# Slots of 384 rows instead of 256, one block of the first layer per PSUM bank in a ring of three, sum of mixture 2 and weight splits behind the fifth block

## What is computed

```python
out = np.einsum('hk,bskhg->bshg', w, x_unf)      # causal 7-tap average per head
# mixture 1: every token goes to its best expert of 8
expert_idx = np.argmax(x @ w_gate, axis=1)
for e in range(E):
    mask = expert_idx == e
    h = np.maximum(x[mask] @ w1[e], 0.0)         # 192 -> 1024
    out[mask] = gate_w[mask, None] * (h @ w2[e]) # 1024 -> 192
# mixture 2: noisy logits, every token goes to two experts of 8
noisy_logits = logits + np.log1p(np.exp(x @ w_noise)) * noise
top2 = np.argpartition(-noisy_logits, 2, axis=1)[:, :2]
for e in range(E):
    for k in range(2):
        mask = top2[:, k] == e
        out[mask] += top2_w[mask, k, None] * (np.maximum(x[mask] @ w1[e], 0.0) @ w2[e])
```

## Time and profile before

| | us |
|---|---|
| median of 3 runs | 2036.11 (2036.06 to 2037.99) |
| the profiled execution, its own time | 2038.28 |
| the profiled execution, its span in the trace | 2036.5 |
| mean granted TensorE clock | 0.978 of 2.4 GHz |
| first matmul of layer 1, mixture 1 | 209.87 |
| first matmul of layer 1, mixture 2 | 874.95 |
| first matmul of layer 1, last slot | 2017.95 |

### The profile page before, as it was taken

How to read it: one execution, slowest core, us unless ns; L and a number is a source line. 1 busy time by engine, 2 the same in 40 slices (tenths; PEclk the granted TensorE clock), 3 DMA queues, 4 the chain that set the end, 5 groups by cost and what they waited for, 6 DMA issues and landing times.

```text
span 2036.5 us, 49899 instructions
## 1 busy us (share of the span) xinstructions
PE 1908.1 (94%) x14519; PEld 1853.4 (91%) x14520; DVE 1216.6 (60%) x4101; ACT 847.5 (42%) x2019; POOL 942.5 (46%) x1174
## 2 busy tenths in 40 slices
PE   7990899999999999789999999999999999999998
PEld 4760899999999999789999999999999999999998
DVE  6551677777777777745555554545555554555554
ACT  2430454444454444433443443433433433434333
POOL 4777244444444444434444444444444444444444
PEclk9995899999999999989999999999999999999999
DMA  6642332332332323222222232221322222312221
GB/s 224 205 158 76 102 113 86 113 113 82 112 102 91 111 86 106 72 92 62 64 89 61 66 91 65 85 74 60 99 61 62 93 62 65 98 60 78 79 63 48
DMA packets 113044, 184.90 MB, mean 91 GB/s; under 512 B 21516, under 2 KB 89092, under 8 KB 110848
## 3 DMA queue, kind: packets, MB, share of 16 engines
q1 hardware_dynamic: 72576, 104.32, 16.8%
q0 software_dynamic: 40320, 79.90, 12.0%
q10 hardware_dynamic: 128, 0.46, 0.1%
HBM read 111.73 MB, written 76.97 MB: 93 GB/s over the span
## 4 chain that ended last, share of the span: by engine, by line
PE 52%; DMA 2%; issue 1%; DVE 1%; POOL 0%; POOLq 0%; DVEq 0%; ACT 0%; ACTq 0%; SPq 0%
PE bank L998 17%; PE bank L999 8%; PE bank L983 5%; PE bank L979 5%; PE bank L980 5%; PE bank L981 5%; PE bank L982 5%; DMA so_far<-out,at_n 1%; PE bank L966 1%; PE bank L968 1%; DMA out<-y,at_c 1%; DVE y L720 0%; DVE y L713 0%; DVE h_l L724 0%; POOL out L1150 0%
## 5 line engine op out<-in xcount | busy, mean ns | idle before, releaser
L998 PE MATMUL bank<-w2hl,h_h 128*128 128x384 f32 (+1 forms) x2832 | 859.6, 368 | 20.3 <-DVE h_l L724 20.3
L999 PE MATMUL bank<-w2hl,h_l 128*128 128x192 f32 (+1 forms) x2832 | 720.3, 254 | 0.0
L998 PEld LDWEIGHTS bank<-w2hl,h_h 128*128 128x128 f32 x2832 | 532.3, 188 | 25.8 <-DVE h_l L724 24.8
L724 DVE SCALAR_TENSOR_TENSOR h_l<-bank,h_h 128x512 fp32r<-128x512 f32 x708 | 468.1, 688 | 138.5 <-ACT h_h L472 119.4
L999 PEld LDWEIGHTS bank<-w2hl,h_l 128*128 128x128 f32 x2832 | 541.6, 191 | 0.0
L472 ACT ACTIVATE h_h<-bank 128x512 fp32r<-128x512 f32 x708 | 421.6, 596 | 277.3 <-PE bank L983 277.2
L979 PE MATMUL bank<-x_h,w1mh 128*128 128x256 f32 x1416 | 402.8, 284 | 3.4 <-DVE x_h L684 3.4
L983 PE MATMUL bank<-x_h,w1ll 128*128 128x256 f32 x1416 | 402.1, 284 | 0.0
L980 PE MATMUL bank<-x_l,w1mh 128*128 128x256 f32 x1416 | 399.5, 282 | 0.0
L982 PE MATMUL bank<-x_h,w1lh 128*128 128x256 f32 x1416 | 399.2, 282 | 0.0
L981 PE MATMUL bank<-x_h,w1ml 128*128 128x256 f32 x1416 | 399.0, 282 | 0.0
(11 more groups left out here) (185 smaller groups left out, 1927.8 us busy)
## 6 DMA issues: line engine op xcount, KB each, us to landing
rows<-rows_of_mixture SPq DMA_DIRECT2D x179, 208.0 KB, 2.6
raw<-in_w_of_both SPq DMA_DIRECT2D x17, 1024.0 KB, 6.3
raw<-in_w_of_both SPq DMA_DIRECT2D x17, 768.0 KB
x_in<-in_x SPq DMA_DIRECT2D x16, 768.0 KB, 4.7
out<-zeros SPq DMA_DIRECT2D x61, 192.0 KB
rows_of_mixture<-row,pos POOLq DMA_INDIRECT x244
rows_of_mixture<-pad_rows SPq DMA_DIRECT2D x18, 208.0 KB, 2.1
so_far<-out,at_n POOLq DMA_INDIRECT x232, 2.8
```

Of the source, the lines that this page charges most:

```text
L724: V.scalar_tensor_tensor(h_l[:, 2 * p:2 * p + 2, :].rearrange("p c t -> p (c t)"), bank[1 + p][:], 0.0, h_h[:, 2 * p:2 * p + 2, :].rearran ...
L998: T.matmul(dst, h_h[:, c, tok], both, start=(c == 0), stop=False)
L999: last = T.matmul(bank[5 + a][:, 0:width], h_l[:, c, tok], w2hl[:, c, 0:width], start=False, stop=(c == F // P - 1))
```

## The change

- A slot has 384 rows in three groups of 128. Layer 1's matmuls have 384 columns, so one block fills a bank. The eight blocks go round three banks (2, 3, 4): block c may start when `relu_l` of block c - 3 has read its bank (the new wait on hl_ready). The turned rows take banks 0 and 1, layer 2's results banks 5, 6 and 7, and the rank matmuls of the routing a bank of the ring.
- ReLU and its low part work on one block (384 columns) at a time, eight times a slot instead of four times 512.
- `weigh_y` signals each of its three groups, and `finish_y` waits for them one by one.
- In mixture 2 adding so_far moves from the end of a slot to behind `relu_l` of the fifth block of the next one (`add_so_far`); the store of a slot waits for that (`summed`).
- The splits of the second layer's weights move behind the fifth block of an expert's first slot, under an If in the loop; the splits of the next first-layer weights go behind blocks 5 to 8 of the last slot. The routing steps move behind the fifth and sixth block.
- To find room in SBUF, raw1, rows, y_b and y2 lie where x_in was; so the load of the first w1 waits for the last convolution. The number of slots is now ceil(n/384), got by a multiplication and a shift (four more small operations in `tables`). Zeros are written in larger pieces.

```diff
-SLOT, SUBS = 256, 2
+SLOT, SUBS = 384, 3
...
+LANES = F // P
+H_BANKS = 3
+ZEROED = 4
...
+RANK_LANE, RANKS_AFTER = 5, 2
...
+        arena = sb("arena", [P, XIN * CHUNK * D])
+        x_in = arena[:].rearrange("p (q t d) -> p q t d", q=XIN, d=D)
...
+        raw1 = in_arena(0, [2, F])
+        rows = in_arena(2 * F, [SUBS, ROW + DL])
+        y_b = in_arena(2 * F + SUBS * (ROW + DL), [SUBS, WY])
+        y2 = in_arena(2 * F + SUBS * (ROW + DL + WY), [SUBS, D])
...
             sp_.wait_ge(folded, E)
+            sp_.wait_ge(conv_done[1], CHUNKS)
             load_w1(0)
...
                 def split_x(s):
-                    act.wait_ge(xt2_done[m], s + 1)
-                    nc.scalar.activation(x_h[:], bank[0][:], ACT.Copy).then_inc(xh_ready[m], 1)
+                    for k in range(2):
+                        act.wait_ge(xt2_done[m], 2 * s + k + 1)
+                        nc.scalar.activation(x_h[:, k * SLOT:(k + 1) * SLOT], bank[k][:, 0:SLOT], ACT.Copy).then_inc(xh_ready[m], 1)
...
                     for a in range(SUBS):
                         scale = meta_c[:, a, GATE:GATE + 1] if m == 0 else w_c[:, a:a + 1]
-                        last = nc.scalar.activation(y_b[:, a, 0:width], bank[5 + a][:, WY:WY + width], ACT.Copy, scale=scale)
-                    last.then_inc(yb_ready[m], 1)
...
+                        nc.scalar.activation(y_b[:, a, 0:width], bank[5 + a][:, WY:WY + width], ACT.Copy,
+                                             scale=scale).then_inc(yb_ready[m], 1)
+
+                def relu(s, c):
+                    act.wait_ge(l1_done[m], LANES * s + c + 1)
+                    nc.scalar.activation(h_h[:, c, :], bank[2 + c % H_BANKS][:, 0:SLOT], ACT.Relu).then_inc(hh_ready[m], 1)
...
-                    for p in range(PAIRS):
-                        split_w2_h(E * m + e, p)
...
+                        if c == 4:
+                            with act.If(at_first < 1):
+                                for p in range(PAIRS):
+                                    split_w2_h(E * m + e, p)
+                            if m == 0:
+                                keep_y(s)
+                        if last and c >= 4:
+                            split_w1_h(E * m + e + 1, c - 4)
...
-                def finish_y(s, link):
-                    dve.wait_ge(yb_ready[m], s + 1)
+                def finish_y(s):
...
                     for a in range(SUBS):
+                        dve.wait_ge(yb_ready[m], SUBS * s + a + 1)
...
+                def add_so_far(s):
+
+                    dve.wait_ge(y_ready[1], s)
+                    dve.wait_ge(so_far_in, 16 * SUBS * s)
+                    V.tensor_tensor(y[:, :, 0:D], y[:, :, 0:D], so_far[:], ALU.add).then_inc(summed, 1)
+
+                def relu_l(s, c):
+                    dve.wait_ge(hh_ready[m], LANES * s + c + 1)
+                    V.scalar_tensor_tensor(h_l[:, c, :], bank[2 + c % H_BANKS][:, 0:SLOT], 0.0, h_h[:, c, :],
...
+                    for c in range(LANES):
+                        relu_l(s, c)
+                        if c == 4:
+                            with dve.If(at_first < 1):
+                                if m == 0:
+                                    split_w2_gates(e, bass.ds(e, 1))
+                                for p in range(PAIRS):
+                                    split_w2_l(E * m + e, p)
+                            if m == 0:
+                                add_noise(s, link)
+                                find_two(s, link)
+                            else:
+                                add_so_far(s)
+                        if c == 5 and m == 0:
+                            mark_two(s, link)
+                        if last and c >= 4:
+                            split_w1_l(E * m + e + 1, c - 4)
...
+                def layer1(s, e, c):
+                    if c == 0:
+                        pe.wait_ge(xl_ready[m], s + 1)
+                    if c % 2 == 0:
+                        pe.wait_ge(w1_ready, PAIRS * (E * m + e) + c // 2 + 1)
+                    if c >= H_BANKS:
+                        pe.wait_ge(hl_ready[m], LANES * s + c - H_BANKS + 1)
...
+                    dst = bank[2 + c % H_BANKS][:, 0:SLOT]
...
+                    for c in range(LANES):
+                        layer2(s, e, c)
+                        if m == 0 and c == RANKS_AFTER:
+                            pe.wait_ge(hl_ready[m], LANES * s + RANK_LANE + 1)
                             second_ranks(s)
...
-                    (y_ready[1], s),
+                    (summed, s + 1),
...
-                    (y_ready[1], s + 1),
+                    (summed, s + 2),
```

More of the change, by code:

```diff
@@ L514, in _ @@
                     start, more = slots_of(act, m, e)
-                    for p in range(PAIRS):
-                        split_w2_h(E * m + e, p)
                     with act.If(more > 0):
                         with act.Fori(0, more) as j:
-                            body(start + j, e, False)
-                    body(start + more, e, True)
+                            body(start + j, e, j, False)
+                    body(start + more, e, more, True)
                 if m == 0:
@@ L801, in body @@
                         place(s, link)
-                    finish_y(s, link)
+                    finish_y(s)
                     dve.wait_ge(y_ready[m], s + 1)
@@ L956, in _ @@
                     pe.wait_ge(r_pos_ready, total + 1)
-                    T.matmul(bank[6][:, 0:E], ones_b[:], count2[:, 0, :], start=True, stop=False)
-                    T.matmul(bank[6][:, 0:E], ones_b[:], count2[:, 1, :], start=False, stop=True).then_inc(counted[m], 1)
+                    for a in range(SUBS):
+                        last = T.matmul(bank[6][:, 0:E], ones_b[:], count2[:, a, :], start=(a == 0), stop=(a == SUBS - 1))
+                    last.then_inc(counted[m], 1)
                 else:
```

170 lines of the change are left out of this document (72 added, 98 removed).

## The result

The changed kernel takes 2122.39 us, the median of 4 runs (2119.97 to 2126.93); the kernel before takes 2036.82 beside it (2036.06 to 2037.99). The ratio is 1.0422, with a 95% interval of 1.0404 to 1.0441: slower by some 85 us. The profiled execution has a span of 2120.0 us where before had 2036.5, so the traces have 83.5 us to explain.

What follows compares the result with a forecast made beforehand. TensorE, its matmul row busy 94% of the span, was taken as the bound. From 2036.5 us, +31.6 and -0.7 (slots), +75 (ring), -12.8 (edges) and +8.5 (fixed parts) gave 2138 us, range 2085 to 2170.

Steps and rivals of the forecast that it cites:

- ring wait: Layer 1's block 4 waits 0.61 to 0.62 us per slot for relu_l to free its bank: 75 us more over 121 slots.
- fixed parts: Extra scatters behind mixture 1, one more store at the end, longer first and last pieces: 8.5 us more.
- edges of experts: At experts' first and last slots, 42.2 us of old waits go, 16.4 and 13 us come or stay: 12.8 us less.
- slots without waits, mixture 2: 80 slots of 14.59 us on TensorE, 1167.2 us together: 31.6 us more than before.
- slots without waits, mixture 1: 41 slots of 15.10 us on TensorE, 619.1 us together: 0.7 us less than before.
- Padding and layer 1 with 384 columns: 41 and 80 slots, mixture 2 computing 3.4% more rows; layer 1's matmul takes 175 ns, bounds 163 to 179.
- A slot without waits: TensorE's layer 1, transposes and layer 2 together take 14.59 us in mixture 2 and 15.10 in mixture 1.
- The sign that was named: On TensorE the fourth block's first matmul starts about 3.1 to 3.3 us into each slot, after idling for VectorE's h_l.
- the loop's way back: On VectorE, 0.46 us of registers and two branches ahead of a slot's first relu_l, said to stay after the change.
- No wait in the ring: Rival, 12%: the first bank is released before 2.47 us into the slot, so no wait; 2047 us at 175 ns.
- Every block waits: Rival, 6%: five blocks of layer 1 wait 0.1 to 0.3 us each, 60 to 120 us more, about 2220.
- The splits starve layer 2: Rival, 3%: w2 comes 1.3 us late for layer 2 at 16 first slots, giving 2159 us.

Runs made afterwards that it cites:

- Experiment 2: The addition of so_far moved back to the end of a slot, before the next first relu_l, in mixture 2 of the changed kernel: 2135.37 us, ratio 1.0471.
- experiment 3: The changed kernel with three banks, without VectorE's wait for its own y at a slot's end (wait, and w_c in mixture 2, moved later): 2060.51 us, ratio 1.011.
- Experiment 4: The changed kernel with the addition of so_far moved ahead of the weight splits, both behind the fifth block, in mixture 2: 2112.88 us, ratio 1.0371.

## Why the prediction was right, and where its terms were off

The direction, the mechanism and its place were right. The time forecast was 2138 us, 16 more than measured, inside the range. Part of the miss cancelled, which was luck: the slots, the ring wait and the fixed parts were put too high by some 24 us together, the edges of experts too low by 6 to 7. The time of a run is also 2 us above its span, where the prediction took it 0.4 below. The ledger, on spans:

| term | predicted | measured | from |
|---|---|---|---|
| slots without waits, mixture 2 | +31.6 | +26.0 | 80 x 14.52 - 1135.6 |
| slots without waits, mixture 1 | -0.7 | -1.1 | 41 x 15.09 - 619.8 |
| ring wait and edges of experts | +62.2 | about +51 | what is left of 83.5 |
| fixed parts | +8.5 | +7.3 | start +0.5, change-over +3.6, end +3.2 |
| sum | +101.6 | +83.5 | 2120.0 - 2036.5 |

**Padding and layer 1 with 384 columns.** The padding was right: 41 and 80 slots. The matmul was predicted at 175 ns; it is 173 to 176 from start to start. The block from 1241.62 on shows it: its fifth matmul starts at 1242.32, four steps of 175 ns later. The Trainium skill (TensorE: Matmul & The Clock Gate, Wait — 56ns, not 53.3ns?) gives N/2.4 + 2.5 ns for a warm matmul, an estimate of 162.5 ns here; the trace does not agree at this size either.

**A slot without waits.** 14.59 and 15.10 were predicted, 14.52 and 15.09 measured with five banks. The 0.07 us in mixture 2 are 5.6 us over 80 slots, most of what this term is off by.

**The ring wait.** The prediction had the release at 3.08 and the question at 2.47, so 0.61 to 0.62. It was 3.02 and 2.50: 0.52 on the weight load, 0.49 in slot time in mixture 2 and 0.45 in mixture 1. The sign that was named, the fourth block at 3.1 to 3.3 us, was missed by 0.08. Over 121 slots 0.13 to 0.17 us are 16 to 20 us, the largest error of the sum. It comes from small ends: y was done at 1.73 instead of 1.79, the matmuls asked 0.03 later, and mixture 1 was taken to be like mixture 2. The stretch from y's end to relu_l came out as summed, 0.68 us against 0.69: the 0.39 us of "issue" are less than the 0.46 of before, but w_c starts 0.12 behind y, where it started 0.03 behind the addition. What was wrong here is not the number but what the prediction says of this stretch: "this is the loop's way back (registers and two branches), and it stays". It does not simply stay. Experiment 2 hid it under the addition, and experiment 3 took it away with the self-wait. This is the mechanism of the rival *No wait in the ring*, "because the 0.46 us of the loop's way back shrink", and it is real; the change as made leaves the sequencer waiting for its own y, so it did not come true. The time that this rival gave at 175 ns, 2047, is that of the kernel with five banks, 2045.89.

**The other rivals.** Blocks 5 to 8 follow without a wait, from 1243.83 on one block in 0.87 us, so *Every block waits* did not come; ReLU took 492 ns and relu_l 555 for 384 columns. *The splits starve layer 2* did not come either: layer 2's first load is not in the list of waits.

**The edges of experts.** Three parts. First slots: the entry of VectorE was priced at 16.4 us above the usual wait, and of the 83.9 us of waits for h_l 24.3 lie in 14 first slots, 17.3 more than 14 regular waits would be (0.5 each). That was right. The mask in mixture 1: 13 us were kept, and about 5 stayed, the 3.2 us for h_l and 1.7 of "issue" ahead of the rank matmuls (L1040). The waits that go: 42.2 us were taken off, but 4.6 of them, the "longest" in the row of the mask in the earlier trace rows, is the one at the change-over between the mixtures, which stands unchanged in the new list. Only 37.6 could go. I misread a row's last number. Not foreseen at all was the second slot of mixture 2, 16.45 us against 15.01, 11.5 us over eight. The prediction costed the move of the sum as a gain in front of relu_l and did not ask what the sum, put behind the splits, makes late: y's store, and through it the y of the next slot. Experiment 4 shows that this is the cause: the sum ahead of the splits takes these 11.5 us out of the second slots, some 3 us of two stretches at half clock among them (last section). The starts of the slots give the term as a whole. Before, the slots at the edges of experts were longer than regular ones by 41 us in sum. In the changed kernel the first ones are 25 us longer (17.47 for 15.54 and 16.22 for 15.01), the second ones of mixture 2 11.5 longer and the last ones 2 shorter (15.40 and 14.87), 35 in sum. So it was about -6, where -12.8 was predicted, and with the ring wait (57 us) this makes the 51 that are left.

**Fixed parts.** 8.5 predicted, 7.3 measured.

**Why longer slots gain nothing here.** Longer slots save nothing that pays for padding: a matmul of layer 1 costs 174 ns for 384 columns, against 118.7 for 256, so per row it is 2% cheaper, and mixture 2 computes 3.4% more rows. Layer 2, transposes and ranks go with the rows. Slots cost about 25 us more and fixed parts 7, which leaves the edges of before, 38 us by the waits and 41 by the slots, as the only thing to win. With five banks and the best order (2036.05 us) they are nearly all won and cancel the rest: it is level with the kernel before. With three banks and the self-wait the ring adds some 60 to 80 us on top.

## What to carry to other kernels

When a ring of buffers gets shorter, find the first release of a pass and write down its whole chain, the sequencer's waits included: here a wait of VectorE for its own result, which orders nothing that the next operation needs, cost 62 us in 121 passes, with the small copy behind it in mixture 2. Do not add up what the sequencer does and what the engine does: here an addition of 0.76 us with its 0.20 of wait cost only 0.24 a slot, since the way back ran under it. An operation moved behind others takes with it every transfer that waits for its result, so ask which buffer that transfer holds. And read the granted clock behind every wait that you make longer: of two of these kernels' losses it makes some 12 and 18 us.

## What the hardware showed that I had not expected

- The way back of a loop costs VectorE 0.39 us in front of relu_l when its queue is empty, and nothing when an operation of 0.76 us is running (relu_l 0.07 after the start of w_c). At an expert's entry, with a load of the slot count, it is 1.48 us of "issue" (in the kernel with 256 rows and the splits moved).
- The last store of the first slot is issued at 1203.87, beside the load of w2 at 1204.74, and y, which waits for it, starts at 1208.88: about 5 us from issue to landing.
- After the 1.82 us of idle time at 1211.25 TensorE's granted clock fell for a short stretch. Busy time by window; the last three numbers are the granted clock, the DMA share and GB/s:

```profile
1212.00:1215.00 3.00, 3.00 (x12) 3.00 (x11) 0.99 (x3) 0.98 (x2) 1.39 (x3) 0.52 0.26 70
1216.00:1224.00 8.00, 8.00 (x58) 7.96 (x57) 2.94 (x7) 1.97 (x5) 5.59 (x6) 1.00 0.32 92
```

0.52 of full speed is the lower of the two levels, 1.2 GHz. The blocks that start at 1212.32 and 1213.92 took 1.60 us each instead of 0.87, so the stretch cost about 1.5 us. A second one lies at 1519, behind the same kind of idle time. The regular ring waits of 0.52 us are not followed by one: over the slot at 1239.83 the granted clock is 1.00. The length of the wait alone does not decide: on the weight load the two waits were 2.14 and 2.55 us, and one of 2.07 at 279.7 was followed by none; where ScalarE signals once, four of seven waits of 2.24 to 2.25 were. With the splits back at the head all 14 of 2.97 to 4.52 were. In the kernel with the sum ahead of the splits it is 1.00 from 1150 to 1300 and from 1450 to 1600, so neither stretch is there; that kernel has one of its own at 694, behind a wait of 2.13 us in mixture 1.
